# Attention and two feed-forward layers on one core: where the inverse sums are spread, how far the first layer lags its pair, and how the first pair is fetched

## What is computed

```python
# attention: q, k, v (2, 8, 576, 64)
scores = q @ k.T / 8                        # per batch and head
keep only scores >= the 32nd largest of a row
attn = softmax(kept) ; x = attn @ v         # -> (1152, 512)
# first layer, w_a, w_b (512, 1536), w_out (1536, 512)
x = ((x @ w_a) * (x @ w_b)) @ w_out
# second layer: 4 experts, w1 (4, 512, 1024), w2 (4, 1024, 512)
out = sum over e of p[:, e] * (relu(x @ w1[e]) @ w2[e])   # p: probs over their row sum
```

## Time and profile before

| what | value |
|---|---|
| median of 3 runs | 860.14 us (859.70 to 860.29) |
| the profiled execution's own time | 860.66 us |
| its span | 858.9 us |
| PE busy | 816.5 us (95%), 5048 instructions |
| DVE busy | 450.9 us (53%) |
| ACT busy | 380.7 us (44%) |
| POOL busy | 309.2 us (36%) |
| granted clock of PE over the span | 0.98 |

### The profile page before, as it was taken

How to read it: one execution, slowest core, us unless ns; L and a number is a source line. 1 busy time by engine, 2 the same in 40 slices (tenths; PEclk the granted TensorE clock), 3 DMA queues, 4 the chain that set the end, 5 groups by cost and what they waited for, 6 DMA issues and landing times.

```text
span 858.9 us, 13220 instructions
## 1 busy us (share of the span) xinstructions
PE 816.5 (95%) x5048; PEld 717.8 (84%) x5048; DVE 450.9 (53%) x892; ACT 380.7 (44%) x701; POOL 309.2 (36%) x273
## 2 busy tenths in 40 slices
PE   4577999989999999999989999999999999999998
PEld 2456888868888888888879899899898898998997
DVE  4999998887999999997022221122121121221221
ACT  2777876756767676767444011230032110230110
POOL 0789874544555555556431000440006100440000
PEclk9967999989999999999999999999999999999999
DMA  9360746483545653546758700220003200000000
GB/s 233 85 193 10 272 135 235 146 237 104 182 140 184 239 189 136 176 143 194 271 201 289 270 1 1 98 98 0 1 1 101 96 1 1 0 1 37 13 25 37
DMA packets 71614, 102.58 MB, mean 119 GB/s; under 512 B 32512, under 2 KB 48896, under 8 KB 71552
## 3 DMA queue, kind: packets, MB, share of 16 engines
q1 hardware_dynamic: 68912, 99.12, 35.1%
q10 hardware_dynamic: 2640, 2.62, 1.0%
HBM read 88.36 MB, written 13.37 MB: 118 GB/s over the span
## 4 chain that ended last, share of the span: by engine, by line
PE 85%; DVE 6%; DMA 3%; POOL 2%; issue 2%; ACT 2%; SPq 1%; ACTq 0%; POOLq 0%
PE ps L576 23%; PE ps L596 23%; PE ps L501 15%; PE ps L486 8%; PE ps L454 4%; PE ps L425 4%; PE ps L434 3%; DVE m L846 2%; DVE work L853 2%; PE ps L463 2%; DMA wo<-wo_d 1%; PE ps L469 1%; DVE work L841 1%; DVE m L838 1%; DMA k_tail<-k_in 1%
## 5 line engine op out<-in xcount | busy, mean ns | idle before, releaser
L744 ACT ACTIVATE h_hi<-ps 128x384 fp32r<-128x384 f32 x96 | 47.0, 490 | 271.1 <-PE ps L576 270.9
L846 DVE MAX8 m<-work 128x8 f32<-128x576 f32 x216 | 153.5, 757 | 0.0
L1001 POOL TENSOR_TENSOR w_lo<-w_raw,w_hi 128x2048 fp32r<-128x2048 f32 x12 | 55.2, 4632 | 254.2 <-ACT w_hi L740 254.2
L886 DVE SCALAR_TENSOR_TENSOR h_lo<-ps,h_hi 128x384 fp32r<-128x384 f32 x96 | 53.3, 558 | 164.6 <-ACT h_hi L744 164.6
L576 PE MATMUL ps<-x_hi,w_hi 128*128 128x384 f32 x384 | 129.0, 336 | 0.0
L576 PE MATMUL ps<-x_hi,w_lo 128*128 128x384 f32 x384 | 128.9, 336 | 0.0
L576 PE MATMUL ps<-x_lo,w_hi 128*128 128x384 f32 x384 | 128.8, 335 | 0.0
L953 POOL TENSOR_TENSOR p_sb<-s_sb,p_sb 128x576 f32<-128x576 f32 x72 | 100.8, 1422 | 56.2 <-ACT p_sb L657 56.2
L596 PE MATMUL ps<-w_hi,h_hi 128*128 128x512 f32 x288 | 112.2, 390 | 0.0
L596 PE MATMUL ps<-w_hi,h_lo 128*128 128x512 f32 x288 | 112.1, 389 | 0.0
L596 PE MATMUL ps<-w_lo,h_hi 128*128 128x512 f32 x288 | 112.0, 389 | 0.0
(11 more groups left out here) (84 smaller groups left out, 1513.5 us busy)
## 6 DMA issues: line engine op xcount, KB each, us to landing
wo<-wo_d SPq DMA_DIRECT2D x96, 512.0 KB, 4.9
w_raw<-moe_w_in SPq DMA_DIRECT2D x16, 1024.0 KB, 6.8
wo_d<-wo SPq DMA_DIRECT2D x12, 512.0 KB, 4.9
wo_raw<-moe_w_out_in SPq DMA_DIRECT2D x12, 256.0 KB, 4.0
v_sb<-v_in SPq DMA_DIRECT2D x18, 128.0 KB, 3.3
w_raw<-moe_w_b_in SPq DMA_DIRECT2D x3, 768.0 KB, 4.6
x_d<-x_hi_out SPq DMA_DIRECT2D x9, 256.0 KB, 2.8
x_d<-x_lo_out SPq DMA_DIRECT2D x9, 256.0 KB, 3.4
```

Source lines behind the costliest of these rows:

```text
L744: copy(h_hi[:, m, :], ps[:, UP + m % FREE_UP, 0:GN], ACT.Relu).then_inc(ac_r, 1)
L846: nc.vector.max(m8[:, par, i, 8 * r:8 * r + 8], work[:, i, :]).then_inc(ve_top, 1)
L886: nc.vector.scalar_tensor_tensor(h_lo[:, m, :], ps[:, UP + m % FREE_UP, 0:GN], 0.0, h_hi[:, m, :].bitcast(F32), ALU.max, ALU.subtract).the ...
L1001: nc.gpsimd.tensor_tensor(lo[:, s, :], raw[s][:], hi[:, s, :].bitcast(F32), ALU.subtract).then_inc(done, 1)
```

## The change

**Inverse sums through DRAM.** `inv_transpose`, `inv_out` and `x_out` are gone. SP stores the 128 x 8 reciprocals to a new DRAM tensor inv_d, transposed, element by element, waits for it, and loads each head's row back to 64 partitions of inv_b (`spread_inverses`). DVE multiplies straight from PSUM (`scale`) and makes xT_lo (`x_low`). `sums` moves behind the second operation of the top-k of the pass, `scale` behind the tenth and `x_low` behind the eleventh; for the first tile the three places are the eighth of pass 4, and the fourth and sixth of pass 5.

**Lag five.** LAG_AB is 5: `up` of a tile's first piece runs in the same pass as its scaling. `h_transpose` stays one pass behind `up`, and `send` comes two passes behind it, at the start of the pass. The transposes of the probabilities move between the two halves of `up`.

**First pair alone.** The tail keys and the queries of the first two heads are fetched and transposed first, the other heads' later; SP, no longer ACT, issues the first three weight slices, behind all keys.

**Around it.** The low part of x2 moves from DVE to POOL, from a second copy that ACT makes; weight slices are split in passes 0 to 4, chunks in 6 to 9; the raw ring of chunks has 5 entries; second-batch keys use other banks and are spread over passes 11 to 14; q and v loads stand behind the reloads in SP's list; the expert weights' first halves are copied in two passes instead of one.

```diff
-        LAG_AB = 6
-        KEYS1 = {11: ("tail", 0), 12: (1, 2), 13: (3,)}
+        LAG_AB = 5
+        KEYS0 = PR + 2
+        KEYS1 = {11: ("tail", 0), 12: (1,), 13: (2,), 14: (3,)}
...
-        SLICES_IN = {1: (0, 1), 2: (2,), 3: (3, 4), 4: (5,), 5: (6, 7)}
-        CHUNKS_IN = {6: (0, 1, 2), 7: (3,), 8: (4, 5, 6), 9: (7, 8, 9), 10: (10, 11)}
+        SLICES_IN = {0: (0, 1), 1: (2,), 2: (3, 4), 3: (5, 6), 4: (7,)}
+        CHUNKS_IN = {6: (0, 1, 2, 3), 7: (4, 5), 8: (6, 7, 8), 9: (9, 10, 11)}
...
+            def spread_inverses(t):
+                sp.wait_ge(ve_den, 2 * t + 2)
+                sp.dma_start(inv_d[t].rearrange("h p -> p h"), x_inv[:],
+                             allow_slow_non_contiguous=True).then_inc(st_inv, 16)
+                sp.wait_ge(st_inv, 16 * (t + 1))
+                if t:
+                    sp.wait_ge(ve_xu, t)
+                for side in range(2):
+                    src = inv_d[t].rearrange("(r z) p -> z r p", z=2)[side].partition_broadcast(D)
+                    dst = inv_b[side * D:(side + 1) * D, :].rearrange("p (r n) -> p r n", r=PR)
+                    sp.dma_start(dst, src).then_inc(ld_inv, 16)
...
             load_k(0, 0, ld_k[0])
             load_k(0, 1, ld_k[0])
-            load_k_tail(0)
-            for pr in range(1, PR):
+            load_k_tail(0, 0, 2, ld_kt[0])
+            load_k(0, 2, ld_k[1])
+            load_k(0, 3, ld_k[1])
+            load_k_tail(0, 2, H, ld_kt_rest)
+            for pr in range(2, PR):
...
+            for i in range(RAW):
+                load_slice(i)
...
             def slot_loads(n):
...
+                if n and finished_tile(n - 1) is not None:
+                    keep_x2(finished_tile(n - 1))
+                u = sent_of(n)
+                if u is not None:
+                    for g in range(FC * u + RING, FC * (u + 1) + RING):
+                        if FO <= g < FC * NP:
+                            reload_chunk(g)
...
+                if scaled_tile(n + 1) is not None:
+                    spread_inverses(scaled_tile(n + 1))
...
-            def inv_transpose(t):
-                pe.wait_ge(ve_den, 2 * t + 2)
-                for h in range(H):
-                    mm = nc.tensor.matmul(ps_a[h % 2 * D:(h % 2 + 1) * D, h // 2 * P:(h // 2 + 1) * P],
-                                          x_inv[:, h:h + 1].to_broadcast([P, D]), ident[:], start=True, stop=True)
-                mm.then_inc(pe_i, 1)
...
+            def scale(t):
+                dve.wait_ge(pe_x, PR * (t + 1))
+                dve.wait_ge(ld_inv, 32 * (t + 1))
+                if t >= 2:
+                    dve.wait_ge(st_x2, 32 * (t - 1))
+                nc.vector.tensor_tensor(xu[:], ps_x[:, :], inv_b[:], ALU.mult).then_inc(ve_xu, 1)
+
+            def x_low(t):
+                dve.wait_ge(ac_xT, t + 1)
+                if t >= 2:
+                    dve.wait_ge(pe_b, PR * (t - 1))
+                nc.vector.tensor_tensor(xT_lo[:, t % 2, :, :], xu[:].rearrange("p (c t) -> p c t", c=DK),
+                                        xT_hi[:, t % 2, :, :].bitcast(F32), ALU.subtract).then_inc(ve_xT, 1)
+
+            SUMS, SCALE, LOW = 2, 10, 11
+            FIRST_SUMS, FIRST_SCALE, FIRST_LOW = 8, 4, 6
```

More of the change, by code:

```diff
@@ L319, in slot_loads @@
                     keep_chunk(g)
+                if next_q(n) is not None and next_q(n) + 1 < NT:
+                    sp.wait_ge(pe_q, next_q(n) + 2)
+                    load_q(next_q(n) + 1)
                 if n == 8:
@@ L331, in slot_loads @@
                         load_w_half(0, 0, s)
[L332 to L344, removed]
+            for n in range(LAST + 2):
                 slot_loads(n)
@@ L389, in keys_pair, with keys_tail, q_transpose @@
                 tr.then_inc(pe_k, 1)
[L391 to L394, removed]
+            def keys_tail(b, pairs):
+                bank = ps[:, 1, :] if b else ps_y
+                for pr in pairs:
+                    tr = nc.tensor.transpose(bank[:, pr * KL:(pr + 1) * KL], k_tail[b][0:KL, pr * P:(pr + 1) * P],
                                              ident[0:KL, 0:KL])
                 tr.then_inc(pe_k, 1)
-            def q_transpose(t, bank):
-                pe.wait_ge(ld_q, 32 * (t + 1))
-                for pr in range(PR):
+            def q_transpose(pairs, bank):
+                for pr in pairs:
                     tr = nc.tensor.transpose(bank[:, pr * P:(pr + 1) * P],
@@ L598, in expert_down @@
                 mm.then_inc(pe_dn, 1)
+            send(NP - 2)
             h_transpose(NP - 1)
@@ new lines, in _, with between @@
+            SUMS, SCALE, LOW = 2, 10, 11
+            FIRST_SUMS, FIRST_SCALE, FIRST_LOW = 8, 4, 6
+            def between(n, done):
+                t = scaled_tile(n)
+                if n == PR and done == FIRST_SUMS:
+                    sums(0)
+                if t is not None and t > 0 and done == SUMS:
+                    sums(t)
+                if t is not None and done == (SCALE if t else FIRST_SCALE):
+                    scale(t)
+                if t is not None and done == (LOW if t else FIRST_LOW):
+                    x_low(t)
@@ L900, in _ @@
                 if n < NP:
-                    top_scores(n, lambda: extras(n))
-                else:
-                    extras(n)
+                    top_scores(n)
+                if n == NP:
+                    sums(NT - 1)
+                if n == NP + 1:
+                    scale(NT - 1)
+                    x_low(NT - 1)
                 if n == NP + 1:
@@ L913, in _ @@
                         nc.vector.tensor_tensor(pr_n[:, :, e], pr_raw[:, :, e], pr_inv[:], ALU.mult).then_inc(ve_pr, 1)
-                if n == NP + 2:
-                    for s in range(2):
-                        low(w1_raw, w1_hi, w1_lo, s, ve_w1, ac_w1)
-            for m in range(3):
+                if n in (NP + 2, NP + 3):
+                    low(w1_raw, w1_hi, w1_lo, n - NP - 2, ve_w1, ac_w1)
+            for m in range(4):
                 hidden_low(0, 0, m)
-            x2_low(NT - 1)
-            hidden_low(0, 0, 3)
             for s in range(2):
@@ L960, in hidden_low, with product, x2_low @@
                 nc.gpsimd.tensor_tensor(hT_lo[:], hT_raw[:], hT_hi[:].bitcast(F32), ALU.subtract).then_inc(po_hl, 1)
+            def product(u):
+                pool.wait_ge(ac_a, u + 1)
+                pool.wait_ge(ac_b, u + 1)
+                if u:
+                    pool.wait_ge(pe_h, u)
+                nc.gpsimd.tensor_tensor(h_sb[:], a_sb[:], b_sb[:], ALU.mult).then_inc(po_h, 1)
+            def x2_low(t):
+                pool.wait_ge(ac_z, 2 * t + 2)
+                nc.gpsimd.tensor_tensor(x2_lo_out[:], xu[:].rearrange("p (c t) -> p c t", c=DK),
+                                        x2_hi_out[:].bitcast(F32), ALU.subtract).then_inc(po_x2, 1)
             for n in range(LAST + 1):
-                t, j, m, u = scaled_tile(n), pair_of(n), unit_of(n), sent_of(n)
+                j, u = pair_of(n), turned_unit(n)
                 if j is not None:
                     limits(j)
+                if u is not None:
+                    product(u)
+                if j is not None:
                     push_down(j, 0)
```

341 lines of the change are left out of this document (156 added, 185 removed).

## The result

The changed kernel takes 947.68 us (942.92 to 948.86, four runs), the kernel before in the same session 860.21 (859.70 to 861.38): a ratio of 1.100, 95% interval 1.096 to 1.105. It is 10% slower, 87 us, where 845 us was forecast. The profiled execution has a span of 946.7 us.

A forecast was written before the change was run, and what follows sets the result against it. DVE was taken to bound the start, PE the middle and the experts. Gains of 8.1 (start), 5 (passes 10 to 15), 0 (steady tiles) and 2 (end) sum to 15.1 us off 860.14: 845.0 us, own range 839 to 851, full range 829 to 862.

The forecast's parts named there:

- The trip: Reciprocals through DRAM: store 3.0 us, loads 3.3, 6.9 in all (5.6 to 11.4), so `scale` waits about 1.7 on DVE.
- Every us beyond 6.9 costs PE one us in eight tiles.: At `scale` on DVE: a longer trip reaches PE one for one; the sign turns at 8.8 us.
- The steady tiles without a long store: Tiles from pass 9 on: 1.55 us saved by dropping inverse transposes, about 1.5 lost to late landings; booked at zero.
- The start, 8.1: First pair alone and lag five: pass 10 earlier by 1.5 us, plus 6.6 for a pass saved at the end.
- the saved pass, 6.6: End of the loop: with lag five a last pass holding only `up`, h and `send` goes, 6.6 us.
- the end's 2: End of the loop: weight copies on ACT stand one per pass, not two in a row; 2 us, bounds 0 to 5.
- DVE bounds until pass 9, pass 10 starts at 116.4: Start: DVE's first MAX8 at 10.4, then about 9.65 us per pass; pass 10 at 116.4 instead of 117.87.
- the start doesn't pay: Rival, passes 0 to 9: POOL's low halves of slices and chunks set the pace; 853 us, chance 0.12.
- Passes 10 to 15, 5: Middle passes: waits for `wo` reloads queued behind q and v mostly go; 5 us gained, bounds 0 to 7.
- The round trip is long: Rival at `scale` on DVE: 863 us with a 5.2 us store, 881 with both upper bounds; chance 0.16 for slower.

The follow-up runs named there:

- e8: Changed kernel with reciprocals turned by a PE matmul, stored as 8 rows of 512 bytes, and weight slices copied early on ACT: 855.19 us, ratio 0.995.
- e1: Changed kernel with the reciprocals stored as 128 runs of 32 bytes instead of 1024 single numbers, turning left out: 866.42 us, ratio 1.007.
- e2: Changed kernel without the DRAM trip: PE spreads the reciprocals by eight matmuls, ACT copies them, the rest stays: 857.40 us, ratio 0.997.
- e5: e2's kernel with ACT copying the weight slices of passes 1 to 4 ahead of the score copies: 850.23 us, ratio 0.988.
- e11: e5's kernel with all weight slices redistributed to finish by pass 4 and the first tile's `scale` and `x_low` earlier: 847.82 us, ratio 0.986.
- e9: e5's kernel plus nine stores of reciprocals that nobody reads, differing by tile in spacing and count of 4-byte numbers: 855.26 us.
- e7: Changed kernel with the reciprocals stored as 512 pieces of 8 bytes instead of 1024 of 4, turning left out: 878.59 us, ratio 1.021.
- e6: Changed kernel with the store issued twice, the second into a DRAM tensor nobody reads, SP waiting for both: 938.63 us, ratio 1.091.

## Why the prediction was wrong, step by step

**The trip, the term that failed.** The store was put at 3.0 us with an upper bound of 5.2 from `pr_raw`. It takes 10.0, and DVE's wait at `scale`, forecast at 1.7, is 10.3. The bound was no bound: `pr_raw` is a load, with runs of 16 bytes, and nothing in the trace of before writes single numbers side by side. I named "4-byte pieces are smaller than any seen" and still closed the range at the nearest row. The loads, put at 3.3, landed after 4.0 in the median. The prediction weighed two statements of the Trainium skill, page "DMA: Bandwidth & Descriptors". The rule against a strided last dimension, section "Rules for kernel authors", was the right one to follow. The estimate of 4.0 us for two transfers, from the fixed 2.0 us of the section "Anatomy of one DMA", is far from the 15.05 of the chain, and that section describes transfers that GpSimd issues, not SP. e8's rows come nearer to it: 1.2 us for the store, 0.6 to issue the first load, 2.9 until the second has landed, some 4.7 in all.

**"Every us beyond 6.9 costs PE one us in eight tiles."** The place was right: `scale` on DVE, then `up` on PE, 74.3 us in eight waits. The price was too low. 15.05 less 6.9 is 8.15 us; a pass with a trip lost 21.45 - 11.78 = 9.67 against before, where zero was booked; 2.1 us of it is the lower clock after the stand, for which the sum had no term.

**The steady tiles without a long store.** Zero was about right: in e1, with 3.3 us for the store, passes 16 to 33 are 9.7 us longer than before (206.0 against 196.3), nearly all of it in the two passes of 16.7 and 16.9 in which PE stood over 3 us and its clock fell; the other three take 11.4 to 12.0, as 11.78 before. In e2, with no trip, these passes are 1.5 us shorter than before. (e1's profiled execution is 5 us over the median of its runs, so the two long passes may be rarer than they look.)

**The start, 8.1.** The first MAX8 at 9.76 (10.4 forecast) came, and most of the end: 7.3 us in e2, where the saved pass, 6.6, and the end's 2 were booked. "DVE bounds until pass 9, pass 10 starts at 116.4" failed by itself, without the trip: 129.41 in e2. The step took DVE's steady row as the pace for all of it, and read nothing of ACT's order. 6.6 of these 13.0 us are the slices behind the score copies (e5), 2.9 more their distribution and the first tile's low part (e11); the other 3.5 no run takes apart. From pass 6 on, PE has an `up` in each pass and takes 10.4 to 11.4 us even in e5, not 9.65. The rival "the start doesn't pay", at 853 us, named POOL and was right as to place and sign, though not as to size (it took 3 off the start, and the 5 of passes 10 to 15, which came) nor wholly as to the cause: POOL stood waiting for ACT. It came on top of the other.

**Passes 10 to 15, 5.** 5.8 in e2. Right.

**The rivals.** "The round trip is long" was the case that came, with its place and direction; its worst price, 881 us, took over the wrong bound. By its own line 15.05 us give 845 + 8 x 8.15 = 910; the clock adds some 8 x 2.1 = 17; the start adds the 13.0 of e2, and the first tile's trip, in pass 5, 20.9 - 13.7 = 7.2 (pass 5 here and in e2). That makes about 947, an estimate from these rows. It had a chance of 0.16, against 0.5 for a sum that stood on an unmeasured operation in each of nine tiles.

## What to carry to other kernels

A transfer of a form that the trace doesn't show has no upper bound in it: where a sum hangs on such a wait in every tile, the chance belongs to the unknown, and the transfer is measured alone before the kernel is built on it. If a table has to go through DRAM, it is turned before the store, so that the store writes whole rows; here even then the eight matmuls on PE were 5 us better (e8 and e5). And when an order of work is moved by one pass, read which engine supplies the next one in the passes where all are busy, not only the engine that sets the pace now.

## What was unexpected about the hardware

- Stores of 4-byte pieces to DRAM take 7.9 to 10.5 us when the pieces are neighbours (256 to 1024 of them), 3.7 to 5.1 when they are 512 or 64 bytes apart (1024), from issue to landing in e9. In the kernels' own trips SP waits 10.0 for 1024 dense pieces of 4 bytes, 4.2 for 512 of 8 bytes (e7), 3.3 for 128 of 32 bytes (e1), 1.2 for 8 of 512 bytes (e8). Two dense stores at once take no longer than one (9.2 in e6).
- During such a store the DMA engines are idle (share 0.04, and 0.00 for its last 6.6 us), so a view of their load doesn't show it; only the wait does.
- A stand of 9.39 us brought PE's clock down to the lower level for the next twelve matmuls, and so did stands of 3.27 and 3.49 in e1; one of 1.33 did not.
- A 0.69 us subtraction on DVE took 3.47 while POOL subtracted a slice. The Trainium skill, page "SBUF — State Buffer", section "Who interferes with whom", says that a VectorE instruction with two inputs in SBUF contends with a GpSimd instruction that reads SBUF, and that the order of issue decides which of them is blocked. The trace agrees: POOL's started first and took 3.43, and DVE's, begun 0.51 us later, ended 0.55 us after it.
